# Filter MLP in one pass instead of two, its stores on another queue, and a lagged combine in an FFT convolution

## The reference

```
h_filt = (maximum(pos_emb @ w1, 0) @ w2) * exp(-0.01 * pos)    # filter MLP, (S, 128)
u      = x * v
y      = irfft(rfft(u, 2S) * rfft(h_filt, 2S))[:, :S]          # along S, per channel
x1     = x * y                                                 # 22912 rows of 128
x2     = moe(x1, modality_id, w_gate, modality_bias, w1, w2)   # top-1 of 8 experts, 128 -> 1024 -> 128
out    = moe2(x2, w_gate, w1, w2)
```

## Time and profile before

| | |
|---|---|
| median of 3 runs | 2006.65 us (2002.93 to 2007.62) |
| the profiled execution | 2007.62 us, its span 2005.8 us |
| TensorE (PE) busy | 1821.4 us, 91% of the span |
| VectorE (DVE) busy | 1250.3 us, 62% |
| ScalarE (ACT) busy | 1003.2 us, 50% |
| GpSimd (POOL) busy | 584.0 us, 29% |
| mean granted TensorE clock | 0.947 of full |

### The profile page before, as it was taken

How to read it: one execution, slowest core, us unless ns; L and a number is a source line. 1 busy time by engine, 2 the same in 40 slices (tenths; PEclk the granted TensorE clock), 3 DMA queues, 4 the chain that set the end, 5 groups by cost and what they waited for, 6 DMA issues and landing times. The chain is left out here.

```text
span 2005.8 us, 34901 instructions
## 1 busy us (share of the span) xinstructions
PE 1821.4 (91%) x9634; PEld 1546.8 (77%) x9634; DVE 1250.3 (62%) x3396; ACT 1003.2 (50%) x2185; POOL 584.0 (29%) x603
## 2 busy tenths in 40 slices
PE   8899989979998069999999999992999999999996
PEld 7866786769888058888888888992888888888886
DVE  1879867947677346777777777664555555555542
ACT  4764484423343035555555555541555555555543
POOL 0000000006777711333332222333133333333333
PEclk9999999989788579999999999995999999999998
DMA  6859775879998377777777777874666666666683
GB/s 214 216 145 284 214 211 169 245 216 312 304 315 280 134 260 241 247 247 249 249 248 254 255 252 252 291 256 162 210 222 233 217 212 224 231 223 210 234 302 125
DMA packets 193269, 469.52 MB, mean 234 GB/s; under 512 B 24691, under 2 KB 75455, under 8 KB 192792
## 3 DMA queue, kind: packets, MB, share of 16 engines
q1 hardware_dynamic: 163736, 415.28, 63.5%
q0 software_dynamic: 18688, 35.99, 5.1%
q10 hardware_dynamic: 10752, 17.12, 2.4%
HBM read 366.14 MB, written 105.28 MB: 235 GB/s over the span
## 5 line engine op out<-in xcount | busy, mean ns | idle before, releaser
L1307 DVE SCALAR_TENSOR_TENSOR m_hid<-m_pH,m_hid 128x512 fp32r<-128x512 f32 x784 | 540.5, 690 | 448.1 <-ACT m_hid L1242 442.2
L1242 ACT ACTIVATE m_hid<-m_pH 128x512 fp32r<-128x512 f32 x784 | 470.5, 600 | 532.2 <-PE m_pH L1165 532.0
L1163 PE MATMUL m_pH<-m_xT,m_w 128*128 128x512 f32 (+1 forms) x864 | 346.6, 401 | 9.3 <-DMA m_w<-halves 6.6
L1180 PE MATMUL m_pO<-m_hid,m_w 128*128 128x512 f32 (+1 forms) x864 | 322.7, 373 | 9.8 <-issue 9.8
L1382 POOL DMA_INDIRECT rows<-m_rows,m_idx x196 | 190.5, 972 | 480.8 <-ACT m_rows L1264 413.1
L1165 PE MATMUL m_pH<-m_xT,m_w 128*128 128x512 f32 (+1 forms) x864 | 322.3, 373 | 0.0
L1164 PE MATMUL m_pH<-m_xT,m_w 128*128 128x512 f32 (+1 forms) x864 | 321.8, 372 | 0.0
L1182 PE MATMUL m_pO<-m_hid,m_w 128*128 128x512 f32 (+1 forms) x864 | 321.0, 372 | 0.0
L1181 PE MATMUL m_pO<-m_hid,m_w 128*128 128x512 f32 (+1 forms) x864 | 319.7, 370 | 0.0
L1386 POOL DMA_INDIRECT out_dram<-m_rows,m_token x196 | 190.5, 972 | 425.7 <-ACT m_rows L1264 363.9
L1001 POOL DMA_INDIRECT rows<-oi_rows,oi_idx x192 | 196.7, 1025 | 95.1 <-issue 83.5
(11 more groups left out here) (192 smaller groups left out, 2309.8 us busy)
## 6 DMA issues: line engine op xcount, KB each, us to landing
m_w<-halves SPq DMA_DIRECT2D x216, 1024.0 KB, 7.3
conv_stage<-in_inner_dram SPq DMA_DIRECT2D x92, 256.0 KB, 4.0
inner_back<-conv_stage SPq DMA_DIRECT2D x92, 256.0 KB, 4.0
oi_C<-inner_back SPq DMA_DIRECT2D x32, 728.0 KB
m_x<-rows SPq DMA_DIRECT2D x88, 264.0 KB, 2.7
halves<-m_parts SPq DMA_DIRECT2D x33, 512.0 KB, 9.7
halves<-oi_parts ACTq DMA_DIRECT2D x32, 512.0 KB, 10.4
conv_stage<-in_x_dram SPq DMA_DIRECT2D x32, 384.0 KB, 6.1
```

The costliest lines, as they stand in the source:

```text
L1163: nc.tensor.matmul(out, high, xT[:, s % 2, 0, cols], start=True, stop=False, skip_group_check=skip)
L1180: nc.tensor.matmul(out, high, hid[:, s % 2, c, 0, cols], start=(c == 0 and t == 0), stop=False, skip_group_check=skip)
L1242: nc.scalar.activation(hid[:, s % 2, c, 0, 0:TILE], pH[:, c % HB, 0:TILE], ACT.Relu).then_inc(H_high, 1)
L1307: nc.vector.scalar_tensor_tensor(hid[:, s % 2, c, 1, 0:TILE], pH[:, c % HB, 0:TILE], 0.0, hid[:, s % 2, c, 0, 0:TILE].bitcast(F32), ALU.ma ...
```

## The change

Five things change together:

- The output of the filter MLP is made in one pass, 16 x 4 matmuls of 256 columns for all channels, beside the hidden layer. `weighed` shrinks to two groups, so VectorE also waits for the output matmuls of two groups before. ScalarE copies each group in two instructions, each out of two PSUM banks, which alternate in pairs.
- The four stores of the filter's upper half to `h_d` go from SyncE's queue, in the middle of the MLP, to ScalarE's queue, behind all of its copies.
- `LEAD` of half 0 is 2 instead of 3: a mix stands one chunk later in VectorE's order.
- In the loop over t, `combine(t - 1)` stands behind `multiply(t)` on VectorE.
- The warm-up of the inverse stage is 6 matmuls of 288 columns on `inv`, behind the wait for it, instead of 5 of 384 columns on `consts`, ahead of it.

```diff
-WARM = 5
+WARM = 6
...
-    LEAD = (3, 3)
+    LEAD = (2, 3)
...
-        weighed = flat[:, 2 * FLAT:3 * FLAT].rearrange("p (i c) -> p i c", c=GC)
+        weighed = flat[:, 2 * FLAT:2 * FLAT + 2 * GC].rearrange("p (i c) -> p i c", c=GC)
...
             sp.dma_start(W[:, :], outer_d).then_inc(W_in, 16)
-            sp.wait_ge(h_copied, GROUPS)
-            for i in range(4):
-                at = CHUNKS_H + 2 * i
-                sp.dma_start(h_d[:, 2 * i * CD * ST:2 * (i + 1) * CD * ST],
-                             stage[0:JP, at:at + 2].rearrange("p c w -> p (c w)")).then_inc(h_stored[i], 16)
             for u in range(CHUNKS_U):
                 load_signals(0, u)
...
-            def output(half, i):
-                turn = (1 - half) * GROUPS + i
+            def output(i):
                 pe.wait_ge(win_done, i + 1)
-                if turn >= 4:
-                    pe.wait_ge(h_copied, turn - 3)
+                if i >= 2:
+                    pe.wait_ge(h_copied, 2 * (i - 1))
                 for t in range(GRP):
-                    last = nc.tensor.matmul(pA[0:JP, 1, turn % 4, t * 2 * HD:(t + 1) * 2 * HD],
-                                            weighed[:, i, t * JP:(t + 1) * JP],
-                                            w2s.rearrange("p (e d) -> p e d", e=2)[:, :, half * HD:(half + 1) * HD],
-                                            start=True, stop=True)
+                    last = nc.tensor.matmul(pA[0:JP, 1, i % 2 * 2 + t // 2, t % 2 * 2 * D:(t % 2 + 1) * 2 * D],
+                                            weighed[:, i % 2, t * JP:(t + 1) * JP], w2s, start=True, stop=True)
                 last.then_inc(h_ready, 1)
...
                 if i >= 2:
-                    output(1, i - 2)
-            for i in range(GROUPS):
-                output(0, i)
+                    output(i - 2)
             pe.wait_ge(h_copied, 2 * GROUPS)
...
-            for turn in range(2 * GROUPS):
-                half, i = 1 - turn // GROUPS, turn % GROUPS
-                act.wait_ge(h_ready, turn + 1)
-                nc.scalar.activation(
-                    h[:, half * HD:(half + 1) * HD, :, i * GRP:(i + 1) * GRP].rearrange("p d e t -> p e d t"),
-                    pA[0:JP, 1, turn % 4].rearrange("p (t e d) -> p e d t", t=GRP, e=2), ACT.Copy
-                    ).then_inc(h_copied, 1)
+            for i in range(GROUPS):
+                act.wait_ge(h_ready, i + 1)
+                for eo in range(2):
+                    src = pA[0:JP, 1, i % 2 * 2:i % 2 * 2 + 2].rearrange("p b (t e d) -> p e d b t", t=2, e=2)
+                    nc.scalar.activation(h[:, :, eo, i * GRP:(i + 1) * GRP].rearrange("p d (b t) -> p d b t", t=2),
+                                         src[:, eo], ACT.Copy).then_inc(h_copied, 1)
+            act.wait_ge(h_copied, 2 * GROUPS)
+            for i in range(4):
+                at = CHUNKS_H + 2 * i
+                act.dma_start(h_d[:, 2 * i * CD * ST:2 * (i + 1) * CD * ST],
+                              stage[0:JP, at:at + 2].rearrange("p c w -> p (c w)")).then_inc(h_stored[i], 16)
...
-                nc.vector.scalar_tensor_tensor(weighed[:, i], pA[:, 0, i % 2, 0:GC], 0.0, win[:, i],
+                if i >= 2:
+                    dve.wait_ge(h_ready, i - 1)
+                nc.vector.scalar_tensor_tensor(weighed[:, i % 2], pA[:, 0, i % 2, 0:GC], 0.0, win[:, i],
                                                ALU.max, ALU.mult).then_inc(win_done, 1)
...
-                for t in range(T):
-                    multiply(half, t)
-                    combine(half, t)
+                for t in range(T + 1):
+                    if t < T:
+                        multiply(half, t)
+                    if t >= 1:
+                        combine(half, t - 1)
...
+            pe.wait_ge(inv_in, 16)
...
             for _ in range(WARM):
-                nc.tensor.matmul(pG[:, 0, 0:3 * 128], consts[:, 0:128], consts[:, :], start=True, stop=True,
-                                 skip_group_check=True)
-            pe.wait_ge(inv_in, 16)
+                nc.tensor.matmul(pG[0:JP, 0, 0:3 * JP], inv[:, 0, :], inv[:, :, :].rearrange("k m j -> k (m j)"),
+                                 start=True, stop=True, skip_group_check=True)
             outer(0, 0)
```

More of the change, by code:

```diff
@@ L145, in convolution @@
         win = flat[:, FLAT:2 * FLAT].rearrange("p (i c) -> p i c", c=GC)
-        weighed = flat[:, 2 * FLAT:3 * FLAT].rearrange("p (i c) -> p i c", c=GC)
-        w1s = flat[:, 3 * FLAT:3 * FLAT + 2 * FO]
-        w2s = flat[:, 3 * FLAT + 2 * FO:3 * FLAT + 2 * FO + 2 * D]
+        weighed = flat[:, 2 * FLAT:2 * FLAT + 2 * GC].rearrange("p (i c) -> p i c", c=GC)
+        w1s = flat[:, 2 * FLAT + 2 * GC:2 * FLAT + 2 * GC + 2 * FO]
+        w2s = flat[:, 2 * FLAT + 2 * GC + 2 * FO:2 * FLAT + 2 * GC + 2 * FO + 2 * D]
         h = stage[0:JP].rearrange("p c w -> p (c w)").rearrange("p (d e s) -> p d e s", e=2, s=HS)
```

## The result

The changed kernel takes 2058.3 us (median of 4 runs, 2048.15 to 2061.36) where the kernel before takes 2004.79 (4 runs): ratio 1.0262, 95% interval 1.0218 to 1.0306, so it is slower by 2.6%. The profiled execution took 2052.0 us, its span is 2050.2, against 2007.62 and 2005.8 before: +44.4 in the span. The prediction said 2052. The ratios of the experiments leave out two executions far from all others (8468.7 us of the new warm-up alone, 2683.8 us of the kernel before, at mean clocks of 0.20 and 0.64).

The account below looks back on a forecast made before the run. The prediction took TensorE's columns to bound the loop, VectorE close behind, and evictions on ScalarE and VectorE to hold up the transforms. Sum: 2007.6 + 31 + 13 + 1.5 = 2053, against the median 2052 us; range 2022 to 2072.

Parts of the forecast that it names:

- case A: Whole kernel: the summed terms hold, 2052 us, own range 2039 to 2060; chance 0.55.
- The loop: Loop over t: combine's lag makes the chain span two steps, step 2.48 instead of 2.146 us; +31, ends 23 and 35.
- The starts: Start of each half's loop: I(0) also waits for multiply(1), 1.29 us each; +2.6.
- The transforms of half 0: Before half 0's loop: late signals and low clock +8, LEAD 2 +4.8; together +13, ends 8 and 16.
- strict order: First signal chunk: v's load queues behind all the stores and lands at 66.5 us; T(7) then comes +10.5.
- The MLP: Filter MLP in one pass: columns bound it, nothing gained from half the weight loads; net 0, transforms begin near 48.8.
- WARM: Start of the inverse stage: six matmuls wait for inv, first outer matmul 0 to 2.4 us late; +1.5.
- B: Signal loads slip between the stores before 57.7; only LEAD's 4.8 stays of the 13: 2044 us; chance 0.13.
- C: Loop over t: the lag costs nothing, the step stays 2.15 us: 2022 us; chance 0.12.
- F: B and C together, signals in time and a lag that costs nothing: 2014 us; chance 0.05.
- E: Loop over t: VectorE sets the step, the lag removes its waits, step 1.92, -19: 1998 us; chance 0.03.
- D: Loop over t: TensorE's idle gaps make the clock fall, +17 to +34: 2070 to 2087 us; chance 0.12.

Follow-up runs that it names:

- LEAD 4: The kernel before with only LEAD = (4, 3) instead of (3, 3), each mix of half 0 one chunk earlier in VectorE's order: ratio 1.0023.
- the lag alone: The kernel before with only combine(t - 1) put behind multiply(t) on VectorE: ratio 1.0134.
- the MLP alone: The kernel before with only the one-pass filter MLP and its stores on ScalarE's queue behind all copies: ratio 1.0066.
- the lag with more room: The kernel before with combine(t - 1) behind multiply(t), and inverse and back_out at t - 3 instead of t - 2: ratio 1.0046.

## Why the prediction was right

The total was right (2052 against 2058.3, and 2052.0 in the profiled execution; +45.5 against +44.4 in the span), and so was its likeliest case A. The parts measured alone add up: 1.34 (lag) + 0.23 (LEAD) + 0.66 (MLP and stores) + 0.37 (warm-up) = 2.60%, against 2.62% for the whole; each has an interval of 0.2 to 0.4 either way, so that they agree to 0.02 is chance. That the total came so close is luck too: three terms were off (the loop 7.5 too high, the transforms of half 0 2.8 and the warm-up 5.9 too low), and their errors cancel. What was no luck is the direction and that the loop is the largest term.

- **The loop.** Predicted +31 (ends 23 and 35), measured +23.5. The mechanism was right: a chain from F to I over two steps. The term was mis-sized in three places. The chain was taken as 4.04 + 0.87 + 0.10, with up to 0.15 off because combine no longer waits for its own multiply. The rows have 0.12 off (3.92 from 344.17 to 348.09), and the 0.10 for weights that can't load ahead is in it (0.97 behind the stalled inverse, 0.86 behind the other). So the step is (3.92 + 0.97)/2 = 2.445, not 2.48, and over 84 steps that is 25.1 instead of 28.1. The starts were to cost 1.3 each and cost nothing: I(0) already came 6.72 us after F(0) in half 0, its first forward matmuls being at half clock, and comes 6.69 after; in half 1 it went from 7.03 to 5.31, as the clock happened to be higher. With that clock full it comes 4.81 after F(0) without the lag (LEAD 4, half 0) and 5.31 with it, so the true price of a start is 0.5, and a beginning at half clock hides it. The tails and the matrices' waits would have to make up the rest; they were not measured by themselves. (The prediction's tail is added up wrong by 0.1: 4.04 - 0.07 + 2 x 0.87 is 5.7, not 5.8.)
- **The transforms of half 0.** Predicted +13 (ends 8 and 16), measured +15.8 up to F(0), the -0.9 of the MLP included. v was taken to land at 64 and VectorE got it at 65.95, near the 66.5 of strict order, far from the minimum of 57.4; T(4) came 8.1 late where 6.1 was said. From T(4) to F(0) it is 70.17 us against 62.52, +7.7, where half clock and LEAD were to give 2.4 + 4.8 = 7.2. The Trainium skill, DMA: Bandwidth & Descriptors, section Queues, rings and completion order, lets the DMA engines take turns between the rings; by that v would have landed near 60. The trace agrees that both queues move data in the same stretch, but from 55 to 59 us the loads had only 0.23 MB of 1.17, and the runs show no gain in time: 17.4 us with two rings, 16.8 with one. The estimate of 60 is refuted by the measurement.
- **The MLP.** Predicted 0, measured -0.9, which is no gain: the first transform comes at 47.25 to 49.15 us in the kernels with the old MLP and at 47.7 to 49.1 in those with the new one.
- **WARM.** Predicted +1.5, measured +7.4. This is the step that failed: "The first outer matmul is 0 to 2.4 late ... It passes straight on". It is 0.7 late; the cost is that the warm-up no longer warms. The prediction priced its matmuls at 1.2 GHz and did not ask at which clock the work behind them would run. Rows that would have raised the question were at hand: outer's 64 records take 7.56 us right behind the old warm-up, and the granted clock there, from 421.6 to 429.1 us, is 1.00.
- **The rivals.** B (signals in time) falls: 7.12 us of wait for v. C and F (the lag costs nothing) fall: a step of 2.44. E falls with VectorE at 70.50 of 88.00. D falls: clock 1.00 in the loop's window, with an idle gap of 0.31 in every second step. The Trainium skill, TensorE: Matmul & The Clock Gate, section on psum-queue depth-cycling, made D likelier; neither this trace nor that of the lag alone (0.99) shows a swing of the clock there.

What stays open: why the transforms of half 1 took 1.6 us less, which the executions without the lag show as well (74.4 to 79.9 us across all runs, without a pattern by edit), and why the loop of half 0 waits for its tables with three steps of lag.

## What to carry to other kernels

In a software pipeline over in-order queues, count how many steps the chain from one engine back to it may span, before and after a reordering: taking one step of slack away costs nothing as long as chain / steps stays below the bounding engine's own step, and afterwards the chain sets the step exactly (4.89/2 here, against 2.146). Here, a store that others wait for cost by the moment at which it left, not by the queue that it was on. A warm-up is judged by the clock of the work behind it, not by the moment at which it ends.

## What the runs showed of the hardware

- The shape of the warm-up decided the clock behind it. After 12 records with 91 x 96 weights and 288 columns (6.04 to 6.08 us, back to back) outer's 64 records took 13.81 to 13.94 us, in 4 of 4 profiled executions, early or late. After 10 records with 128 x 128 weights and 384 columns they took 7.6 to 8.1 us in 7 of 9, and 11.6 and 11.7 in the other two (the MLP alone, and the lag with more room), where the clock fell back: 1.00 from 428.4 to 431.4 us, 0.50 from 434.4 to 441.0 in the first of them. So the old warm-up works, but not each time: gating takes 35.7 us in the MLP's own profiled execution, 4.7 more than before, 4.0 of it in these 64 records. How many of its other executions had this, and so how much of its 0.66%, is not known.
- On another chip the scatters took 303 to 314 us instead of 256 to 262, with 236 instead of 319 GB/s in the 100 us that begin 59 us after the stage does (LEAD 4 there, the kernel before here), and the kernel before 2061.25 us instead of 2002 to 2005. Only the kernel before ran there as well as on the others, so whether ratios carry over was not tested.
